# Weight staging of ten buffers, earlier shifts and low halves on GpSimd between attention and the first tile of a fused attention, Fourier and expert kernel

## What is computed

```python
# attention: batch 4, 8 heads, 576 positions, 64 wide, a window of 128 behind, a slope per head
scores = np.where(mask, scale * q @ k.T + bias, -1e9)
attn = softmax(scores); x = attn @ v                  # joined to rows of 512
# Fourier mixing and an MLP 512 -> 2048 -> 512
mixed = np.real(np.fft.fft(np.fft.fft(x, axis=1), axis=2))
u = x + mixed
un = (u - mean(u)) / np.sqrt(var(u) + 1e-06)
x2 = u + np.maximum(un @ w_ch1, 0.0) @ w_ch2
# eight experts 512 -> 1024 -> 512, one for each row, chosen by a gate and a running rule
out[b, s] = p[e] * (np.maximum(x2[b, s] @ w1[e], 0.0) @ w2[e])
```

## Time and profile before

| | us |
|---|---|
| three timed runs | 900.43, 900.96, 906.88 |
| their median | 900.96 |
| the profiled execution | 899.51 |
| its span, first to last instruction | 897.6 |
| busy: TensorE, VectorE, ScalarE, GpSimd | 844.9, 548.0, 307.4, 272.2 |

### The profile page before, as it was taken

One profiled execution on the slowest core, in us unless ns is written; L12 is line 12 of the kernel. 1 busy time (PEld: TensorE's weight loads), 2 busy tenths in 40 slices (PEclk: granted clock), 3 DMA queues, 4 the chain that ended last, 5 costly groups with the idle time before them and its releaser, 6 DMA issues.

```text
span 897.6 us, 22524 instructions
## 1 busy us (share of the span) xinstructions
PE 844.9 (94%) x8820; PEld 607.7 (68%) x8821; DVE 548.0 (61%) x1125; ACT 307.4 (34%) x461; POOL 272.2 (30%) x287
## 2 busy tenths in 40 slices
PE   8988988799999999999999999939999999999995
PEld 4776777776667676767676767517777777777773
DVE  6899987866757474748483839769995883000000
ACT  5789887543111111111111111103333333333331
POOL 1457878311010101011111100013444444334431
PEclk9999999999999999999999999959999999999998
DMA  9455543458110101010101003405774772111100
GB/s 289 133 176 159 175 144 98 134 184 236 48 48 23 47 23 47 23 47 23 47 23 47 24 24 133 126 27 165 259 236 143 229 234 77 48 45 50 50 24 0
DMA packets 60474, 91.28 MB, mean 102 GB/s; under 512 B 7304, under 2 KB 30971, under 8 KB 60421
## 3 DMA queue, kind: packets, MB, share of 16 engines
q1 hardware_dynamic: 55061, 74.80, 26.9%
q0 software_dynamic: 5360, 15.74, 5.5%
HBM read 73.16 MB, written 16.57 MB: 100 GB/s over the span
## 4 chain that ended last, share of the span: by engine, by line
PE 70%; DVE 11%; DMA 7%; SPq 3%; issue 3%; ACT 3%; POOL 1%; DVEq 0%; POOLq 0%; ACTq 0%
PE psum L926 19%; PE psum L909 19%; PE psum L1102 13%; PE psum L1086 13%; DMA m_mem<-in_qk 2%; DVE arena L1436 1%; DVE m_mem L1408 1%; DMA arena<-in_mlp_w 1%; PE psum L1053 1%; SPq L627 1%; DMA m_mem<-x_rows,m_mem 1%; PE psum L676 1%; DVE arena L1429 1%; ACT psum L1161 1%; PE psum L885 1%
## 5 line engine op out<-in xcount | busy, mean ns | idle before, releaser
L909 PE MATMUL psum<-m_mem,arena 128*128 (+1 forms) x1728 | 197.6, 273 | 0.0
L926 PE MATMUL psum<-arena,m_mem 128*128 128x512 f16 x864 | 195.5, 379 | 0.4 <-DVE m_mem L1590 0.4
L909 PEld LDWEIGHTS psum<-m_mem,arena 128*128 128x128 f16 x1728 | 169.1, 98 | 27.8 <-issue 0.4
L926 PEld LDWEIGHTS psum<-arena,m_mem 128*128 128x128 f16 x864 | 84.5, 98 | 91.1 <-DVE m_mem L1590 0.9
L1086 PEld LDWEIGHTS psum<-m_mem,arena 128*128 x2400 | 137.1, 97 | 7.0 <-issue 1.5
L1086 PE MATMUL psum<-m_mem,arena 128*128 128x128 f16 x2400 | 139.5, 218 | 1.2 <-issue 0.6
L1102 PE MATMUL psum<-arena,m_mem 128*128 x600 | 133.4, 379 | 0.0
L1269 ACT ACTIVATE m_mem<-psum 128x512 f16<-128x512 f32 x72 | 43.0, 597 | 236.1 <-PE psum L909 236.1
L1619 DVE SCALAR_TENSOR_TENSOR m_mem<-m_mem,arena 128x512 f16<-128x512 f32 x144 | 102.8, 768 | 0.0
L1102 PEld LDWEIGHTS psum<-arena,m_mem 128*128 128x128 f16 x600 | 57.6, 98 | 65.2
L2001 POOL TENSOR_TENSOR arena<-m_mem,arena 128x1024 f16<-128x1024 f32 x9 | 19.2, 2138 | 255.1 <-ACT arena L1280 210.4
(11 more groups left out here) (243 smaller groups left out, 1070.0 us busy)
## 6 DMA issues: line engine op xcount, KB each, us to landing
dimdft_sb<-in_exp_w SPq DMA_DIRECT2D x74, 256.0 KB
wstage<-in_exp_w SPq DMA_DIRECT2D x54, 256.0 KB
m_mem<-in_qk SPq DMA_DIRECT2D x16, 576.0 KB, 4.4
arena<-in_v SPq DMA_DIRECT2D x32, 160.0 KB, 2.6
x_rows<-m_mem SPq DMA_DIRECT2D x16, 320.0 KB, 3.0
x_rows<-arena SPq DMA_DIRECT2D x9, 512.0 KB, 2.8
wstage<-in_mlp_w SPq DMA_DIRECT2D x16, 256.0 KB
arena<-in_mlp_w SPq DMA_DIRECT2D x16, 256.0 KB, 4.1
```

The source lines that it names most:

```text
L909: last = nc.tensor.matmul(psum[:, 2 + k % 4, (f % 2) * 2 * P:(f % 2 + 1) * 2 * P], w1_sb[:, sp_, c, f * P:(f + 1) * P], unT[:, bass.ds(t % ...
L926: last = nc.tensor.matmul(psum[:, 6 + q, :], hT[:, k % 4, sp_, at:at + P], w2_sb[:, mp, f, :], start=f == 0 and sp_ == 0 and mp == 0, stop ...
```

## The change

The ring of staging buffers grows from four to ten; the six new ones lie in space that attention no longer uses once item 15 is normalised, and of them five lie where the broadcast gate rows go later. No load of the ring stands ahead of the shift of item 15 any more. Load n waits for the low half of chunk n-10. The folds over columns and the low halves of items 14 and 15 go from VectorE to GpSimd, the second fold and both low halves behind the gather. The low halves of chunks 0 and 1 go from between `normalise(14)` and `normalise(15)` to behind `spectrum_lo(0)`. Nine chunks instead of eleven are split before tile 0, and the order of the pieces changes on ScalarE and VectorE. On SyncE the first two expert chunks go ahead of the gate broadcasts, and the tables go behind these.

```diff
-W_DFT = 7
-W_TILE0 = [3, 3, 4, 3, 4, 4, 0, 0]
+W_DFT = 5
+W_TILE0 = [4, 4, 4, 3, 4, 4, 0, 0]
...
+        W_EARLY = len(w_staging)
+        late_at = [ends_at + 2 * D - 2 * P] + [SLOT_WORDS - 2 * CH * (i + 1) for i in range(5)]
+        w_staging += [arena[:, at:at + 2 * CH].bitcast(F32) for at in late_at]
         WRING = len(w_staging)
...
             shift_x(PAIRS - 2)
             store_x(PAIRS - 2)
-            W_TOP = W_SPEC + W_DFT
-            for n in range(WRING, WRING + 2):
-                load_w(n)
             shift_x(PAIRS - 1)
             store_x(PAIRS - 1)
+            for n in range(W_EARLY, W_EARLY + 3):
+                load_w(n)
...
-            for n in range(WRING + 2, W_TOP + 3):
+            for n in range(W_EARLY + 3, WRING + 9):
                 load_w(n)
...
-            load_w(W_TOP + 3)
             sp.wait_ge(edge_rows, 2)
             sp.dma_start(x_dram[B * SP_ROWS:B * SP_ROWS + B, :], x288[0:B, :]).then_inc(edge_stored, 16)
-
-            for dst, src in ((prefix_sb, prefix), (ids_sb, ids), (iota_sb, iota_e), (negiota_sb, neg_iota),
-                             (reset_sb, reset), (thr_sb, thresholds), (slot_iota, slotiota), (blk_iota, blkiota)):
-                sp.dma_start(dst, src).then_inc(tables_in, 16)
-            sp.dma_start(kiota_sb[0:1], kiota).then_inc(tables_in, 16)
             sp.wait_ge(gateT_copied, 1)
             sp.dma_start(gate_dram, gateT).then_inc(gate_out, 16)
-            for n in range(W_TOP + 4, WCH):
+            for n in range(WRING + 9, WCH):
                 load_w(n)
+            load_exp(0)
+            load_exp(1)
             sp.wait_ge(gate_out, 16)
             for e in range(E + 1):
...
-            load_exp(0)
-            load_exp(1)
+            for dst, src in ((prefix_sb, prefix), (ids_sb, ids), (iota_sb, iota_e), (negiota_sb, neg_iota),
+                             (reset_sb, reset), (thr_sb, thresholds), (slot_iota, slotiota), (blk_iota, blkiota)):
+                sp.dma_start(dst, src).then_inc(tables_in, 16)
+            sp.dma_start(kiota_sb[0:1], kiota).then_inc(tables_in, 16)
```

VectorE:

```diff
             normalise(PAIRS - 2)
-            for n in range(W_SPEC // 2):
-                w_lo_of(n)
             normalise(PAIRS - 1)
...
             spectrum_lo(0)
+            w_lo_of(0)
+            w_lo_of(1)
             dve.wait_ge(middle_clear, 1)
             middle_lo_of(1)
-            w_lo_of(2)
...
-            end_fold_d(PAIRS - 2)
             dve.wait_ge(eo_done, PAIRS)
...
+            w_lo_of(2)
+            spectrum_lo(1, (1,))
+            fold(0, first=True, at=4)
             w_lo_of(3)
+            spectrum_lo(2, (0,))
             w_lo_of(4)
-            spectrum_lo(1, (1,))
-            end_fold_d(PAIRS - 1)
-            fold(0, first=True, at=4)
+            spectrum_lo(2, (1,))
+            moments(0)
             w_lo_of(5)
-            spectrum_lo(2, (0,))
-            end_x_lo(PAIRS - 2)
-            w_lo_of(6)
-            spectrum_lo(2, (1,))
-            end_x_lo(PAIRS - 1)
-            w_lo_of(7)
-            moments(0)
+            normalise_u(0, un_first)
+            spectrum_lo(3, (0,))
             middle_lo_of(2)
-            w_lo_of(8)
-            spectrum_lo(3, (0,))
-            normalise_u(0, un_first)
-            w_lo_of(9)
             spectrum_lo(3, (1,))
             unT_lo_of(0, at=4)
-            w_lo_of(10)
+            for n in range(6, 9):
+                w_lo_of(n)
```

GpSimd:

```diff
             fold_x(PAIRS - 1)
+            fold_d(PAIRS - 2)
             xl_lo_of(B - 1)
             pool.wait_ge(const_in, CONSTS * 16)
...
             nc.gpsimd.memset(xrow_sb[0:1, 0, 1:2], B * SP_ROWS).then_inc(row0_set, 1)
+            fold_d(PAIRS - 1)
+            x_lo_of(PAIRS - 2)
+            x_lo_of(PAIRS - 1)
```

More of the change, by code:

```diff
@@ L543, in _ @@
             load_qk(2, 0)
-            for n in range(4):
+            for n in range(W_EARLY):
                 load_w(n)
@@ L1302, in _ @@
             spectrum_hi(0, (1,))
-            w_hi_of(4)
             x_hi_of(PAIRS - 3)
@@ L1306, in _ @@
             spectrum_hi(1, (0,))
-            w_hi_of(5)
             xl_hi_of(B - 1)
+            x_hi_of(PAIRS - 2)
             spectrum_hi(1, (1,))
             act.wait_ge(m_clear, 1)
+            x_hi_of(PAIRS - 1)
             copy_b(0, first=True, at=4)
-            x_hi_of(PAIRS - 2)
+            w_hi_of(4)
+            spectrum_hi(2, (0,))
+            w_hi_of(5)
+            spectrum_hi(2, (1,))
             w_hi_of(6)
-            x_hi_of(PAIRS - 1)
-            spectrum_hi(2, (0,))
+            std_of(0)
+            spectrum_hi(3, (0,))
+            middle_hi_of(2)
+            spectrum_hi(3, (1,))
             w_hi_of(7)
-            spectrum_hi(2, (1,))
+            unT_hi_of(0, at=4)
             w_hi_of(8)
-            middle_hi_of(2)
-            spectrum_hi(3, (0,))
-            w_hi_of(9)
-            std_of(0)
-            spectrum_hi(3, (1,))
-            unT_hi_of(0, at=4)
-            w_hi_of(10)
             mlp(0, first=True)
@@ L1668, in _ @@
             spectrum_lo(1, (0,))
-            def end_fold_d(n):
-                dve.wait_ge(eo_done, PAIRS)
-                dve.wait_ge(ends_copied, B)
-                dve.wait_ge(x_split, n - 1)
-                nc.vector.tensor_tensor(xd[:, n % 2], xb[:, 2, :, 0:P], xb[:, 3, :, P:0:-1],
-                                        ALU.add if n % 2 == 0 else ALU.subtract).then_inc(d_done, 1)
-            def end_x_lo(n):
-                dve.wait_ge(x_hi, n + 1)
-                nc.vector.tensor_tensor(xparts[:, 1, n].rearrange("p t j -> p (t j)"),
-                                        xd[:, n % 2].rearrange("p t j -> p (t j)"),
-                                        xparts[:, 0, n].rearrange("p t j -> p (t j)"), ALU.subtract)\
-                    .then_inc(x_split, 1)
-            end_fold_d(PAIRS - 2)
             dve.wait_ge(eo_done, PAIRS)
```

## The result

| | before | changed |
|---|---|---|
| median of 20 runs, us | 903.04 | 898.64 |
| lowest, highest | 900.43, 906.88 | 893.79, 901.60 |
| profiled execution, its span | 899.51, 897.6 | 893.79, 892.0 |

The ratio is 0.995, with an interval of 0.9936 to 0.9965: 4.5 us gained, 3.2 to 5.8. That is within 1%, and 898.64 lies in the range of 893.2 to 900.6. But the 0.6 us between forecast and median flatter it. The three runs known at the time had a median of 900.96, and more runs of the same kernel put it at 903.04. The prediction held one per cent for the least that a measurement can tell from no change; the interval tells half a per cent.

A forecast was written before the change was run, and what follows sets the result against it. TensorE was taken as the bound, busy 844.9 of 897.6 us. Gains of 1.0 (Fourier stage) and 1.9 (tile 0) from 899.51 gave 896.6, plus 1.45 for the median 898.0 us; range 893.2 to 900.6.

The forecast's parts named there:

- What bounds the kernel: TensorE, 145 to 232 us: six waits of 7.5 us, plus some 3 us lost at half clock; 10.5 us at most.
- Part 1: Shift of item 15: normalise(15) 1.6 us earlier, TensorE's 0.7 us wait gone, last shift issue 1.2 us earlier.
- part 2: Fourier stage, two folds and two low halves on GpSimd: tile 0 starts at 181.6 instead of 182.62, 1.0 us gained.
- the 0.7: TensorE's 0.7 us wait for normalise(15), claimed to end.
- the turns behind `fold(0)`: VectorE waits for GpSimd's SBUF instructions, up to 1.2 us each; `spectrum_lo(2, 0)` ends at 171.2, TensorE stands still about 5 us.
- The second case: Fourier stage: turns cost little, stand-still 2 us, clock stays up, total gain 5.9 to 7.4, median 894.3 us; chance 0.3.
- the wait of 3 to 6 us: Sign that the forecast holds: TensorE's L839, before spectrum(3,0), waits 3 to 6 us for VectorE's L1515.
- Part 3: Tile 0, staging and queues: TensorE's waits for `un_done(1)` and `hidden_lo` go, 1.9 us gained.
- Both waits: TensorE's tile 0 waits, 1.5 us for `un_done(1)` and 0.4 for the last `hidden_lo`, claimed to go.
- GpSimd did not become the bound: Case denied here: GpSimd's second column fold holds `fold(0)` past 168, tile 0 starts at 185.5, 902.0 us; chance 0.08.
- tile 0 did not keep its waits: Case denied here: loads bound by the queue, the 1.5 us wait stays, gain 1.0 to 1.4, 899.8 us; chance 0.08.
- the 3.7: TensorE's longest wait before the change, 3.7 us for `un_done(0)`, after which the clock fell to 1.2 GHz.

The follow-up runs named there:

- low halves back: Changed kernel with `w_lo` 0 and 1 between normalise(14) and normalise(15) again; ratio 0.9948 against the kernel before.
- copy first: Changed kernel with `copy_b(0)` ahead of the high half of item 15 on ScalarE; ratio 0.9946 against the kernel before.
- chunks 0 and 1 late: Changed kernel with low halves 0 and 1 behind `fold(0)`, three instead of six ahead of `un_done(0)`; ratio 0.9935 against the kernel before.
- ring of four: Changed kernel without the six new staging buffers, order kept; median 902.07 us, ratio 0.9988 against the kernel before.
- changed again: The changed kernel, unedited, run and profiled again on another chip; median 897.36 us, ratio 0.9949 against the kernel before.
- both steps on VectorE: Changed kernel with column folds and low halves of items 14 and 15 back on VectorE, nine chunks; 897.69 us, ratio 0.9939.
- SyncE's old order: Changed kernel with tables before gate rows, gate broadcasts before first expert chunks and waiting for the ring's last low half; 903.85 us, ratio 1.0006.

## Why the prediction was right, and where it was not

**What bounds the kernel: right.** The waits that I named are where the time came from, in tile 0 above all. Part 1 and the first term of part 2, up to `fold(0)`, are on the mark: the 0.7 gone, `fold_x(15)` at 157.4 for 157.8, `fold(0)` at 165.15 for 165.1. But the 0.7 was worth nothing by itself, as the kernel with the low halves back shows. And the shift's gain is not steady: in the profiles with the change or part of it `fold_x(15)` starts 8.1 to 10.5 us after item 15's products (before 10.8), late where it waits for the shift to land, as in copy first (2.3 us).

**The mis-sized term: the turns behind `fold(0)`, in part 2.** I let L1557 wait 1.1, L1558 1.2 and `w_lo` 3 1.1 us. Measured are 0.66 for the first (1.07 less 0.41), nothing for the other two, so `spectrum_lo(2, 0)` came 2.5 us sooner and the wait was 2.05 us, not 5. What failed is the time of the gather, 5.3 us taken from the trace of before, 6.1 here. It decides whether `u_q` finds VectorE in its fold. It is no fixed number: the profiles have 5.3 to 7.3 us, and what sets it is open. The price of a turn was too high too, 0.5 us for L1558's and not 1.2 where the gather was in time (chunks 0 and 1 late). Of the ten profiles with the folds on GpSimd, eight have 1.07 or 1.08 us for the instruction that was L1557. The ring of four alone shows the forecast's course (2.44); with the copy first (2.92) it is the two low halves that hold it. So the mechanism, turns that end in a wait for `spectrum_lo(2, 0)`, was right, and its size was not.

The second case, "the turns cost little", had named this very thing (a slower gather, L1995 missing VectorE's fold, a stand-still of 2 us). It describes this profile's `spectrum_lo(2, 0)` and wait. Counted from item 15's products it had `un_done` at 22.1 to 24.1 us and tile 0 at 28.1 to 30.1; measured are 24.4 and 30.4, just past its late ends. It was wrong to keep the clock at 2.4 GHz, but in this profile the 3.4 us at half clock cost little: from `un_done` to the last low half are 3.86 us, against 3.58 in changed again and in the low halves back, where the clock was up during spectrum(3). That is 0.3 us. The rest of the distance to the case's middle is `un_done`, for which one turn of 0.5 us, `w_lo` 4's, is on record. Of the signs that I had named, the waits that go, the low clock in spectrum(3) and ScalarE without waits for DMA came; the wait of 3 to 6 us and the long L1558 and `w_lo` 3 did not.

That the median lies in the range owes something to luck. The forecast was built on the median of three runs, 2.1 us under that of twenty, and on a gain below the measured interval; the one made up for most of the other.

**What sets tile 0's start.** I had worked it out as `un_done`, then the transposes, then the last low half. In the changed kernel the last low half alone sets it: 2.1 us behind it tile 0 starts if the clock is up (changed: 30.39 less 28.26; low halves back: 30.52 less 28.39), and 3.7 if it is down over `edge` (changed again: 32.34 less 28.60). Before the change it was 4.3 (33.69 less 29.37), for there TensorE was still at its transposes, at half clock. This is why moving the load ahead of `un_done` did so little.

**Part 3, tile 0: right, a little small.** Forecast 1.9, measured 2.45. Both waits are gone, and tile 0 took 44.09 to 44.11 us in eight of the twelve further profiles, against 46.55 before. With both steps on VectorE and with chunks 0 and 1 late it took 1.0 and 1.1 more, because there the half clock reached into the tile. `normalise_u(1)` ended 26.9 us into the tile, where I had some 27. The 0.55 beyond the two waits is in the rows too. Tile 0's first 72 matmuls took 8.17 before and 8.03 after, which is 0.14 of it. And each wait costs more than its record, which counts from the end of the row ahead, while rows without a wait overlap a little. Here are the matmuls ahead of `un_done(1)`, before and after:

```profile
207.80 2.75 PE L926 MATMUL psum<-arena,m_mem 128*128 128x512 f16 x12
```

```profile
204.75 2.75 PE L925 MATMUL psum<-arena,m_mem 128*128 128x512 f16 x12
```

From their start to that of the transposes are 4.26 us before (to 212.06) and 2.59 after (to 207.34): 1.67 us for a wait on record as 1.50. The wait of 0.41 costs 0.59 in the same way. Two edits alone take back more than their intervals leave open, SyncE's old order (1.0006, with its added wait) and the ring of four: 0.9988 without the six buffers and 0.9949 with them, some 3.5 us, of which tile 0 holds 2.0 (46.06 less 44.10) in the profile. Against the twenty runs of the changed kernel the ring's interval, from 0.9968, only just clears theirs, to 0.9965. That the gate broadcasts come later cost nothing: TensorE waits for nothing in the tile.

**The other cases.** GpSimd did not become the bound (`fold(0)` at 165.15, the case needed 168), and tile 0 did not keep its waits. The median lies between the forecast's gain of 2.9 and the second case's 6.7 (900.96 less 894.3), nearer to the forecast.

**What stays open.** How the 4.5 us divide over many executions is open. Tile 0's 2.45 stands in both profiles of the changed kernel (44.10 and 44.11), which leaves some 2 us for the Fourier stage as an estimate; the two profiles of the changed kernel give it 3.3 and 1.35, and which part of the change it comes from no run isolates. Whether the early shift is worth anything by itself was not tried. The time at which item 15's products start differs from 148.9 to 152.5 us over the profiles, as much as the Fourier stage gained; the one profile of the kernel before has the earliest of all, and the cause isn't shown.

## What to carry to other kernels

Where a ring of buffers makes a load wait for the split of the chunk few places before, a deeper ring took out a stand-still, but it lengthens the distance for whatever reuses its space: order the queue's transfers by when they are due, then check that the late one still has slack. Moving work to GpSimd relieves VectorE less where the two read operands from SBUF in the same microseconds: here the move was worth nothing that could be measured. And before pricing a wait, ask which wait ends last behind it. Last, one profile is one execution: the same program gave a stage 30.4 and 32.3 us.

## What the runs showed of the hardware that was not expected

In the Fourier stage the granted clock fell behind a stand-still of 1.9 to 3.4 us in all profiles of kernels with the change or part of it but two (changed: after 2.05; changed again: after 2.48, while it stayed up after 2.06), and in the two not at all (low halves back, with 1.82 and 2.48; copy first, with 2.40 and 2.43). It was low for 3.4 or for 6.8 us. Before the change I had only the 3.7 and took a clean 2 us for safe. A waiting VectorE instruction need not be served after one of GpSimd's: one that takes 0.41 alone took 2.92 us beside two of together 2.77, and 2.44 beside the end of two low halves and the two halves of `u_q`. The Trainium skill ("SBUF — State Buffer", section "Who interferes with whom") calls the shared port pair "an exclusive lock" and says that issue order decides who blocks; the traces agree. I had reckoned with one each. And the gather from its start to its rows took 5.3 to 7.3 us over the profiles, where I had taken one row of 5.3 for its price.
